# One pipeline over all four batches of a sparse attention, with local keys stored in the order of their transposes

## What is computed

```python
B, H, S, D = 4, 8, 576, 64
scores = scale * q @ k.T
mask_local   = (rel >= 0) & (rel < 32)                       # heads 0-3
mask_strided = (rel >= 0) & (pos[None] % 32 == pos[:, None] % 32)   # heads 4-7
attn = softmax(where(mask, scores, -1e9));  x = attn @ v     # x: 2304 rows of 512
out[skip > 0] = x + gate * (relu(x @ w1[e]) @ w2[e])         # e = argmax of x @ w_gate, 8 experts
y = leaky(out @ w_in) @ w_out                                # 512 -> 2048 -> 512
```

## Time and profile before

| what | us |
|---|---|
| median of 3 runs (771.88 to 779.18) | 775.92 |
| the profiled execution | 777.4 |
| its span in the profile | 775.2 |
| attention, to the last `xo` | 156.5 |
| routing | about 45 |
| experts, from the first matmul | 202 to 352 |
| MLP | 352 to the end |

### The profile page before, as it was taken

How to read it: one execution, slowest core, us unless ns; L and a number is a source line. 1 busy time by engine, 2 the same in 40 slices (tenths; PEclk the granted TensorE clock), 3 DMA queues, 4 the chain that set the end, 5 groups by cost and what they waited for, 6 DMA issues and landing times.

```text
span 775.2 us, 12846 instructions
## 1 busy us (share of the span) xinstructions
PE 716.9 (92%) x4628; PEld 664.1 (86%) x4628; DVE 276.2 (36%) x578; ACT 262.0 (34%) x522; POOL 180.5 (23%) x182
## 2 busy tenths in 40 slices
PE   2989979993699999998999999999999999999997
PEld 2878868873699999997999999998989899999986
DVE  4667656757100000003332333233333333332222
ACT  4687666651111112212222223322232322222222
POOL 2120100011686666562100310040031004001000
PEclk9999998986699999999999999999999999999999
DMA  8483746779799999972100210030012004001001
GB/s 175 107 188 100 168 102 171 218 236 229 168 317 341 300 314 338 315 248 64 43 1 0 70 54 1 7 116 1 1 59 63 0 0 122 0 0 41 1 0 41
DMA packets 73112, 91.46 MB, mean 118 GB/s; under 512 B 26704, under 2 KB 47728, under 8 KB 73073
## 3 DMA queue, kind: packets, MB, share of 16 engines
q1 hardware_dynamic: 63969, 66.14, 29.7%
q0 software_dynamic: 8048, 24.79, 11.3%
q10 hardware_dynamic: 1056, 0.02, 0.1%
HBM read 73.91 MB, written 17.01 MB: 117 GB/s over the span
## 4 chain that ended last, share of the span: by engine, by line
PE 74%; SPq 10%; DMA 5%; DVE 3%; issue 3%; ACT 2%; another core or an unknown queue 2%; ACTq 0%; DVEq 0%; POOLq 0%
PE psum L1584 26%; PE psum L1603 26%; PE psum L1497 8%; PE psum L1513 8%; SPq L401 6%; DMA x_rows<-xo 3%; SPq L396 2%; SPq L386 1%; ACT kt L797 1%; PE psum L1336 1%; PE psum L1523 1%; PE psum L1566 1%; DMA x_sb<-x_rows 1%; SPq L409 1%
## 5 line engine op out<-in xcount | busy, mean ns | idle before, releaser
L1584 PE MATMUL psum<-x2h,wih 128*128 128x384 f32 x384 | 130.6, 340 | 1.9 <-DVE x2l L1256 1.9
L1274 DVE SCALAR_TENSOR_TENSOR g_act<-g_raw 128x384 f32<-128x384 f32 x96 | 53.6, 558 | 219.4 <-ACT g_raw L960 205.9
L1584 PE MATMUL psum<-x2h,wil 128*128 128x384 f32 x384 | 129.5, 337 | 0.0
L1584 PE MATMUL psum<-x2l,wih 128*128 128x384 f32 x384 | 129.0, 336 | 0.0
L960 ACT ACTIVATE g_raw<-psum 128x384 f32<-128x384 f32 x96 | 47.2, 492 | 235.3 <-PE psum L1584 232.0
L1603 PE MATMUL psum<-woh,g_l 128*128 128x512 f32 x288 | 114.0, 396 | 0.0
L1603 PE MATMUL psum<-wol,g_h 128*128 128x512 f32 x288 | 113.7, 395 | 0.0
L1603 PE MATMUL psum<-woh,g_h 128*128 128x512 f32 x288 | 112.1, 389 | 0.7 <-DVE g_l L1278 0.7
L1497 PE MATMUL psum<-xt,wring 128*128 128x160 f32 x512 | 80.9, 305 | 0.6 <-issue 0.6
L759 POOL DMA_INDIRECT out_dram<-o_sb,idxo x15 | 15.9, 1061 | 277.8 <-ACT o_sb L955 274.8
L1513 PE MATMUL psum<-hp,wring 128*128 128x160 f32 x512 | 77.6, 299 | 0.0
(11 more groups left out here) (177 smaller groups left out, 899.2 us busy)
## 6 DMA issues: line engine op xcount, KB each, us to landing
wring<-in_moe_w_dram SPq DMA_DIRECT2D x64, 512.0 KB, 8.6
y_rows<-zrow SPq DMA_DIRECT2D x1, 4800.0 KB
q_st<-in_q_dram SPq DMA_DIRECT2D x8, 576.0 KB
k_st<-in_k_dram SPq DMA_DIRECT2D x8, 576.0 KB
x_sb<-x_rows SPq DMA_DIRECT2D x4, 1024.0 KB, 6.4
stage<-in_moe_w_in_dram POOLq DMA_DIRECT2D x4, 1024.0 KB, 9.0
stage<-in_moe_w_out_dram POOLq DMA_DIRECT2D x4, 1024.0 KB, 9.2
vs<-in_v_dram SPq DMA_DIRECT2D x20, 128.0 KB, 7.6
```

Source lines behind the costliest of these rows:

```text
L1274: dve.scalar_tensor_tensor(out=g_act[:, f % 2, :], in0=g_raw[:, f % 2, :], scalar=LEAK, in1=g_raw[:, f % 2, :], op0=ALU.mult, op1=ALU.max) ...
L1584: last = pe.matmul(bank[f % 2][:, 0:MT * P], wt[:, c, f * P:(f + 1) * P], xp[:, T.par, c, :], start=(c == 0 and n == 0), stop=(c == KD - 1 ...
```

## The change

All engines now run one straight sequence over the 44 groups of the four batches, with no hardware loop in the attention, so that the pipeline goes over a batch boundary as it goes over any other step, and all buffers alternate by the running number of the group. Chunks 8 to 15 move to groups 1 to 4, two in each, and chunks 0 to 7 of the next batch stay at groups 7 to 10. DVE copies chunks 9 and 13, and in batch 0 also the odd ones of 0 to 7.

The local keys are kept in `kt` as the transposes leave them: 8 blocks of 76, one for each c. The copies of k chunks 2, 3, 6 and 7 write in order. In exchange the score matmul of a local group reads its 128 moving keys with a step of 76 elements (304 bytes) eight times over, and writes its output in order as before. Queries and strided keys are stored as before.

POOL takes all four copies of q and k for each batch, and for batch 0 those of heads 4 to 7; ACT has none. For batch 0 the heads 0 to 3 are loaded and copied in two halves of two heads, and heads 4 to 7 are loaded after three loads of v. POOL instead of DVE sets the second half of `kt` to zero. ACT no longer waits for the routing weights at the start. In SP's queue q and k of the batch after next are issued as pairs at groups 1 and 6 (before: at groups 2, 4, 6 and 8).

```diff
-        CH_AT = {2: [12], 3: [13], 4: [14], 5: [15], 7: [0, 1], 8: [2, 3], 9: [4, 5], 10: [6, 7]}
-        ON_DVE = {9, 11}
+        CH_AT = {1: [8, 9], 2: [10, 11], 3: [12, 13], 4: [14, 15]}
+        CH_NEXT = {7: [0, 1], 8: [2, 3], 9: [4, 5], 10: [6, 7]}
+
+        def on_dve(b, n):
+            return n % 2 == 1 if b == 0 and n < 8 else n in (9, 13)
...
-                if pr < 2:
-                    lo = STRIDE if kind else 0
+                if pr < 2 and kind:
+                    v_ = t.rearrange("d (c p) -> d c p", c=8)[:, 4 * hf:4 * hf + 4, STRIDE // 8:]
+                elif pr < 2:
+                    lo = 0
                     v_ = t[:, lo:lo + S].rearrange("d (p c) -> d c p", c=8)[:, 4 * hf:4 * hf + 4, :]
...
+            qk_load(sp, 0, 0, q, q_st, s_qs[0], PAIRS[0])
+            qk_load(sp, 0, 0, k, k_st, s_ks[0], PAIRS[0])
+            qk_load(sp, 0, 0, q, q_st, s_q2, PAIRS[1])
+            qk_load(sp, 0, 0, k, k_st, s_k2, PAIRS[1])
             sp.wait_ge(s_vz, 2)
-            for g in range(NL):
+            for g in range(3):
                 v_load(sp, 0, g)
...
+            qk_load(sp, 0, 1, q, q_st, s_qs[1])
+            qk_load(sp, 0, 1, k, k_st, s_ks[1])
+            for g in range(3, NL):
+                v_load(sp, 0, g)
+            qk_next(1, 0)
...
-            def batch(b, qk_ahead, v_ahead):
+            for b in range(B):
                 for g in range(NG):
                     sp.wait_ge(s_xo, NG * b + g + 1)
                     if g in (2, 5) or g >= NL:
                         x_store(sp, b, g)
-                    if v_ahead:
+                    if b + 1 < B:
                         v_load(sp, b + 1, g)
-
-                    if qk_ahead and g in (2, 6):
...
+                    if b + 2 < B and g in (1, 6):
+                        qk_next(b + 2, g // 6)
...
-            act.wait_ge(s_wg, 32)
-            act.activation(wgs[:, :, 0:E + 1], wg[:, :, :], ACT.Copy).then_inc(s_wgh, 1)
...
-                    last = pe.matmul(bk[:, h, :], qt[:, pr, qs], kt[:, h % 2, pr, ks],
-                                     start=False, stop=(h == 3))
+                    keys, to = kt[:, h % 2, pr, :], bk[:, h, :]
+                    if G["local"]:
+                        p0 = G["t"] * QL // 8
+                        keys = keys.rearrange("d (c p) -> d p c", c=8)[:, p0:p0 + P // 8, :]
+                        to = to.rearrange("m (p c) -> m p c", c=8)
+                    else:
+                        keys = keys[:, ks]
+                    last = pe.matmul(to, qt[:, pr, qs], keys, start=False, stop=(h == 3))
...
+            for b in range(B):
+                for g in range(NG):
+                    for n in CH_AT.get(g, []):
+                        chunk(b, n)
+                    for n in CH_NEXT.get(g, []):
+                        if b + 1 < B:
+                            chunk(b + 1, n)
+                    if g in (0, NL):
+                        copied(b, 15 if g else 7)
+                    scores(b, g)
+                    if NG * b + g >= 2:
+                        probs(*divmod(NG * b + g - 2, NG))
+                    if NG * b + g >= 3:
+                        values(*divmod(NG * b + g - 3, NG))
```

More of the change, by code:

```diff
@@ L81, in attention_experts_mlp @@
     ident = at(keep, "ident", [P, P])
+    warm = at(keep, "warm", [P, 1])
     identb = at(keep, "identb", [P, P], BF16)
@@ L216, in attention_experts_mlp @@
         s_zd = sem("s_zd")
+        s_kz = sem("s_keys_zeroed")
+        s_q2 = sem("s_q_second_pair")
+        s_k2 = sem("s_k_second_pair")
         s_qs = [sem("s_qs0"), sem("s_qs1")]
@@ L404, in v_count, with qk_load @@
             return 16 if GROUPS[g]["local"] else 16 * HL
[L406 to L417, removed]
+        def qk_load(eng, b, hs, src, dst, s_, half=slice(0, HL)):
+            h0, h1 = HL * hs + half.start, HL * hs + half.stop
+            eng.dma_start(dst[:, h0:h1, :], src[b:b + 1, h0:h1].rearrange(
+                "o h (p c) d -> p (o h) (c d)", c=8)).then_inc(s_, 16)
@@ L436, in x_load @@
+            qk_load(sp, 0, 1, k, k_st, s_ks[1])
+            for g in range(3, NL):
+                v_load(sp, 0, g)
+            qk_next(1, 0)
+            for g in range(NL, NG):
+                v_load(sp, 0, g)
+            qk_next(1, 1)
             def x_load(b):
@@ L612, in split @@
                 pool.tensor_tensor(lo, src, hi.bitcast(F32), ALU.subtract).then_inc(s_lo, 1)
[L616 to L624, removed]
+            for b in range(B):
+                for hs in range(2):
+                    for dst, src, s_load, s_in in ((q_in, q_st, s_qs[hs], s_qi[hs]),
+                                                   (k_in, k_st, s_ks[hs], s_ki[hs])):
+                        if b == 0 and hs == 0:
+                            continue
+                        if b:
+                            pool.wait_ge(s_tq, len(CH) * (b - 1) + 8 * (hs + 1))
+                        pool.wait_ge(s_load, loaded(b, hs))
+                        carry()
+                        to, what = heads_in(dst, src, hs)
+                        pool.tensor_copy(to, what).then_inc(s_in, 1)
             pool.wait_ge(s_xo, NG * B)
@@ L828, in rest @@
-            def rest(b, last):
-                for s_ in range(2, NG):
-                    for n in CH_AT.get(s_, []):
-                        if n >= 8:
-                            chunk(b, n)
-                        elif not last:
-                            chunk(b + 1, n)
-                    probs_out(b, s_ - 2)
-                    exps(b, s_)
-                    if s_ in (6, 8) and not last:
-                        act.wait_ge(s_tq, len(CH) * b + len(CH))
-                        act.wait_ge(s_qs[1], 16 * b + 32)
-                        to, what = heads_in(q_in, q_st, 1)
-                        h2 = slice(s_ // 8 * 2, s_ // 8 * 2 + 2)
-                        part = act.activation(to[:, :, h2, :], what[:, :, h2, :], ACT.Copy)
-                        if s_ == 8:
-                            part.then_inc(s_qi[1], 1)
@@ L1372, in head @@
-            def head(b):
-                before = not isinstance(b, int)
-                new = b + 1 if before else b
-                for n in (8, 9):
-                    chunk(new, n)
-                if before:
-                    probs(b, NG - 2)
-                    values(b, NG - 3)
-                for n in (10, 11):
-                    chunk(new, n)
-                if before:
-                    probs(b, NG - 1)
-                copied(new, 7)
-                scores(new, 0)
-                if before:
-                    values(b, NG - 2)
-                scores(new, 1)
-                if before:
-                    values(b, NG - 1)
@@ L1393, in rest @@
-            def rest(b, last):
-                for s_ in range(2, NG):
-                    if s_ == NL:
-                        copied(b, 15)
-                    for n in CH_AT.get(s_, []):
-                        if n >= 8:
-                            chunk(b, n)
-                        elif not last:
-                            chunk(b + 1, n)
-                    scores(b, s_)
-                    probs(b, s_ - 2)
-                    if s_ >= 3:
-                        values(b, s_ - 3)
```

268 lines of the change are left out of this document (122 added, 146 removed).

## The result

The changed kernel takes 777.72 us (median of 20 runs, 776.0 to 780.34), the kernel before 773.29 (20 runs, 769.68 to 779.18). The ratio is 1.0055, with an interval of 1.0042 to 1.0068: no change by the bound of 1%, but slower by 4.4 us rather than faster. I had forecast 760 and a range up to 773. What came is the third rival, which I had given 0.15: PE pays for reading its keys by a step. It said 777 us and batches of 34 us.

What follows compares the result with a forecast made beforehand. PE, with 27.5 us of work a batch, was taken to lose 5 to 6 us waiting mainly for ACT's copies. Start -3.5 and batches -2.65, -3.5, -7.45, -0.4 sum to -17.5: 777.4 to 759.9, predicted 760, range 750 to 773.

Steps and rivals of the forecast that it cites:

- the third rival: Local score matmuls: PE pays for stepped reads as ACT does for writes, 0.92 us a group; 777 us, chance 0.15.
- strided reads by PE: Score matmuls of local groups: reading keys with a 304-byte step adds 0, upper bound 0.92 us a group.
- PE's own work: Attention batch: PE's local steps, strided steps, last group and chunks sum to 27.5 us without waits.
- The 2.5 us that I counted: Attention batch: PE's remaining waits for ACT's copies behind groups 2, 4, 8 and 10, making 30.0 us.
- Copies in order: ACT's eight local key copies a batch: 0.42 us each instead of 0.67 when written in order.
- The start: Before group 2 of batch 0: it comes at 23.0 instead of 26.5 us, -3.5; bounds 20.5 and 26.5.
- Batch 2: Attention batch 2: 31.0 instead of 38.45 us, -7.45, with 1 us of the store wait left in.
- The block behind the attention: Everything after the attention: assumed to shift as a block with the attention's end.
- batch 0: Attention batch 0, from group 2 to the next group 2: 30.0 instead of 32.65 us, -2.65.
- the last batch: Attention batch 3, without chunks of a next batch: 25.0 instead of 25.4 us, -0.4.
- The first: Rival on transfers: stores of `xo` wait behind q and k loads; sum -8, 769 us, chance 0.22.
- The second: Rival on ACT's copies: in-order ones are no cheaper, 2 us a batch come back; 764 us, chance 0.08.

Runs made afterwards that it cites:

- e1: The changed kernel with local keys stored by position again, so copies write with a step and PE reads in order: 774.27 us, ratio 1.001.
- e5: e4 with the stores of `xo` issued from ACT's queue, four groups later, instead of SP's: 758.43 us, ratio 0.9795.
- e7: The kernel before, unchanged, run and profiled once more: 774.45 us, one run.
- e6: The kernel before with only the chunk copies walked in destination order, so that they write runs: 773.31 us, ratio 0.9997.
- e4: e1 with all chunk copies writing runs and reading PSUM by a step: 771.17 us, ratio 0.9961.
- e3: The changed kernel with local score reads stepping 8, 16 or 64 bytes or in runs of 16 keys, by batch: 773.65 us, one run.
- e8: The changed kernel with 32 more semaphore increments on PE between attention and routing: 774.79 us, one run.
- e11: The changed kernel with only the stores of `xo` moved to ACT's queue: 783.03 us, ratio 1.0099.

## Why the prediction was wrong

**The step that failed: strided reads by PE, "I take 0".** Measured are 0.88 us a local group, beside my upper bound of 0.92 from ACT's stepped writes.
**PE's own work.** 27.5 us a batch plus 6 x 0.88 is 32.8; PE is busy for 33.4 of 34.7, and of the other 1.3 it waits 1.2 for ACT. The 2.5 us that I counted beside free reads were never put to the test by themselves: e1 has free reads and 4.5 us of waits for ACT in batch 1, but its local key copies take 0.66 us and not 0.41; e5 has 1.1 us of them and batches of 29.5, but its strided key copies are cheap too.

**Copies in order, 0.42 us.** Right: four such copies on ACT take 1.66 us in one piece, where four stepped ones in the earlier trace rows take 2.77.

```profile
76.52 1.66 ACT L816 ACTIVATE kt<-psum 64x288 f32<-64x288 f32 x4
```

**The start, -3.5 us.** Better than forecast: group 2 comes at 20.95, 5.5 us earlier and near my lower bound of 20.5.

**Batch 2, -7.45 us.** Over a third of my sum came from one wait with its low clock. It comes in some executions and not in others: that batch takes 31.8 us in e7, and 37.77 with the wait in e6. My base was high with it: 777.4 against a median of 773.3 over 20 runs, 4 us of my sum that no step of the change could give.

**The block behind the attention** does not shift as one: against the profile before, the end of the attention is 0.6 us earlier, the routing takes 2.7 less, the stretch from the first matmul of the experts to the first of the MLP 2.8 more (3.2 of it behind the experts' last matmul), and the MLP 1.8 more (from 360 to 363 us its clock is 0.50, before 1.00). Together that is the span's +1.3.

**The rivals.** The third came true in its mechanism, with 34.64 us a batch for its 34 and 0.88 us a group for its 0.92. That its 777 met 777.7 is luck twice over. The start (2 us early), batch 0 (1.9 long), the batches 1 and 2 (0.6 each) and the last batch (1.2 short) cancel out. And it was reckoned from the high base: from the median it would have been 0.6 us faster, 772.7, where the change is 4.4 slower. The first, stores behind loads, was real but waited behind it: it costs most once PE is near 30 us a batch (e4, and e6 from the kernel before). So even with free reads my 760 would have needed the stores moved: e4, free reads and cheaper copies than I had assumed, gives 771.17. Whether 760 would come with the stores moved and my copies as assumed has no run. The second, dearer in-order copies, is out.

**What it takes.** From e5, stepped reads give back 14.4 us, stepped copies 14.9, and stores on SP 12.7 (e4; a part of that is a clock of 0.961 to 0.973 there, against 0.971 to 0.982). Each alone uses up nearly the whole gain of 16, since any one of PE's reads, ACT's copies and the stores holds the kernel at 771 to 773 us. (The runs compared stand on three chips, on which the kernel before takes 773.7 to 774.5.) What the new order alone is worth stays open: no run has the old order with copies in runs and the stores on ACT's queue. The change eased ACT a little and loaded PE by more.

## What to carry to other kernels

When a layout is chosen, let the engine that fills the buffer write in runs (16 bytes were enough here) and read PSUM by a step, and do not hand a TensorE that is the bound a float32 moving operand with one element to 16 bytes; where a price is unknown and the nearest row gives one, take that row's, not zero. Before a stall in one profiled execution becomes a term of the sum, look whether the execution is typical of the runs. When several engines are near each other in work, ask what a batch takes if only one is eased, and expect next to nothing from any edit that stands alone.

## What the runs showed of the hardware

- PE reads float32 moving columns with a step of 8 bytes nearly as fast as in order (1.08 us for eight instructions of 128, against 1.04), and with 16, 64 or 304 bytes at close to half (1.99, 1.90, 1.92). The Trainium skill, "Advanced Engine Details and Errata", section "SBUF Cachelines", asks for at least two hits on a 16-byte line; e3 agrees to the step.
- ACT copies 288 elements from PSUM in 0.40 us when it writes runs of four or more and reads by a step, and in 0.66 when it writes by a step. Only the write side counted (e1 against e4).
- A gap of 2.4 us in PE's instructions, with nothing to wait for, was gone with 32 more instructions ahead of it (e8, one execution).
- PE busy throughout, but at the lower clock for some 6.5 us of a batch, cost 2.2 us of it, in the two steps that grew (e11, batch 1). Why the clock falls in some executions and not in others (e7, batch 0), and after one stop and not after the same one in another batch (e11), stays open.
